# Top-32 attention and a Mish MLP in fp32: four engine programs turned from slots of one duo into rounds of four duos

## What is computed

```python
# q, k, v: (4, 8, 576, 64); w_in: (512, 2048); w_out: (2048, 512)
scores = scale * np.matmul(q, k.transpose(0, 1, 3, 2))
kth = np.partition(scores, -32, axis=-1)[..., -32:-32 + 1]
scores = np.where(scores >= kth, scores, -1000000000.0)
scores = scores - np.max(scores, axis=-1, keepdims=True)
attn = np.exp(scores)
attn = attn / (np.sum(attn, axis=-1, keepdims=True) + 1e-09)
x = np.matmul(attn, v).transpose(0, 2, 1, 3).reshape(2304, 512)
h = x @ w_in
y = (h * np.tanh(np.log1p(np.exp(h)))) @ w_out      # Mish, with h cut at 20 in the exponent
```

## Time and profile before

| what | value |
|---|---|
| median of 3 runs (lowest, highest) | 774.0 us (773.94, 775.21) |
| profiled execution: its time, its span | 774.75 us, 773.0 us |
| busy in the span: PE, DVE, ACT, POOL | 718.6, 700.3, 583.5, 547.0 us |
| longest instructions in sum | DVE `topk` MAX8 L574, 432 of 751 ns; PE `up` L388, 2304 records of 279 ns |
| DMA | 34.64 MB, mean 45 GB/s |

### The profile page before, as it was taken

One profiled execution on the slowest core, in us unless ns is written; L12 is line 12 of the kernel. 1 busy time (PEld: TensorE's weight loads), 2 busy tenths in 40 slices (PEclk: granted clock), 3 DMA queues, 4 the chain that ended last, 5 costly groups with the idle time before them and its releaser, 6 DMA issues.

```text
span 773.0 us, 16774 instructions
## 1 busy us (share of the span) xinstructions
PE 718.6 (93%) x6280; PEld 642.3 (83%) x6280; DVE 700.3 (91%) x1513; ACT 583.5 (75%) x1026; POOL 547.0 (71%) x677
## 2 busy tenths in 40 slices
PE   3266699999999999999999999999999999999998
PEld 2255688988888888888888888898899888888986
DVE  6999999999999999999999999999999999999000
ACT  5676677878787878888888888877888888887521
POOL 3877677798777777788777777778777777776531
PEclk9998989999999999999999999999999999999999
DMA  9521000031121000110110000011122000000000
GB/s 341 195 63 35 8 8 12 28 86 59 51 86 51 22 8 22 39 45 16 56 43 21 8 23 8 29 45 52 42 90 77 22 8 22 8 18 2 15 1 28
DMA packets 22689, 34.64 MB, mean 45 GB/s; under 512 B 2384, under 2 KB 11600, under 8 KB 22096
## 3 DMA queue, kind: packets, MB, share of 16 engines
q1 hardware_dynamic: 22608, 33.56, 13.3%
HBM read 28.84 MB, written 4.72 MB: 43 GB/s over the span
## 4 chain that ended last, share of the span: by engine, by line
PE 55%; DVE 35%; POOL 4%; issue 3%; ACT 3%; DMA 0%; SPq 0%; ACTq 0%
PE ps_u L388 22%; DVE left L566 17%; PE ps_y L401 16%; DVE top L574 13%; PE ps_s L329 5%; PE ps_s L347 5%; DVE top L559 5%; PE ps_o L372 5%; PE ps_o L365 1%; POOL g_lo L611 1%; POOL p_sb L625 1%; POOL p_sb L636 1%; ACT p_sb L472 1%; ACT L472 0%; ACT k_hi L432 0%
## 5 line engine op out<-in xcount | busy, mean ns | idle before, releaser
L574 DVE MAX8 top<-left 128x8 f32<-128x576 f32 x432 | 305.3, 751 | 0.0
L388 PE MATMUL ps_u<-xT,win 128*128 128x128 f32 x2304 | 276.6, 279 | 2.5 <-ACT xT L489 2.5
L388 PEld LDWEIGHTS ps_u<-xT,win 128*128 128x128 f32 x2304 | 264.9, 193 | 13.0 <-issue 8.4
L566 DVE MATCH_REPLACE8 left<-top,left 128x576 f32<-128x576 f32 x288 | 212.5, 749 | 0.0
L625 POOL TENSOR_TENSOR p_sb<-x_sb,p_sb 128x576 f32<-128x576 f32 x144 | 200.9, 1417 | 0.0
L472 ACT ACTIVATE p_sb<-p_sb,neg_max 128x576 f32<-128x576 f32 x144 | 110.7, 773 | 24.0 <-POOL p_sb L625 23.5
L453 ACT ACTIVATE x_sb<-ps_s 128x576 f32<-128x576 f32 x144 | 85.7, 648 | 46.1 <-PE ps_s L329 46.1
L401 PE MATMUL ps_y<-w_hi,g_hi 128*128 128x512 f32 x288 | 119.5, 415 | 0.0
L401 PE MATMUL ps_y<-w_hi,g_lo 128*128 128x512 f32 x288 | 113.1, 393 | 0.0
L401 PE MATMUL ps_y<-w_lo,g_hi 128*128 128x512 f32 x288 | 112.4, 390 | 0.0
L636 POOL TENSOR_SCALAR p_sb<-p_sb,recip 128x576 f32<-128x576 f32 x144 | 106.2, 749 | 8.3 <-DVE recip L549 8.0
(11 more groups left out here) (41 smaller groups left out, 823.5 us busy)
## 6 DMA issues: line engine op xcount, KB each, us to landing
v_sb<-v_in SPq DMA_DIRECT2D x32, 320.0 KB, 3.9
g_raw<-w_out SPq DMA_DIRECT2D x8, 512.0 KB, 3.9
win<-w_in SPq DMA_DIRECT2D x4, 1024.0 KB, 12.8
y_out<-y_sb SPq DMA_DIRECT2D x16, 256.0 KB, 2.0
k_raw<-k_in SPq DMA_DIRECT2D x14, 288.0 KB, 3.0
q_raw<-q_in SPq DMA_DIRECT2D x60, 64.0 KB, 1.8
q_raw<-q_in SPq DMA_DIRECT2D x8, 128.0 KB, 2.0
p_sb<-k_in SPq DMA_DIRECT2D x2, 288.0 KB, 5.3
```

The lines of the kernel that those rows point to most:

```text
L388: mm = pe.matmul(ps_u[:, n % 2, i, :], win[:, k, P * f:P * f + P], xT[:, k, :], start=(k == 0), stop=(k == KC - 1), skip_group_check=True)
L566: dve.match_replace(out=left[:, t, :], in_to_replace=best[:, t, EIGHT * r:EIGHT * r + EIGHT], in_values=x[t] if r == 0 else left[:, t, :], ...
L574: dve.max(best[:, t, EIGHT * r + EIGHT:EIGHT * r + 2 * EIGHT], left[:, t, :]).then_inc(found, 1)
```

## The change

Every engine's loop now runs over rounds of four duos, m from -2, with all steps of a round written out. In round m stand the steps of the duos 4m+4 to 4m+7 from `penalty` on, and both the whole `up` and the whole `down` of block m. The list differs from the slots in these points:
- block m's `down` stands in the same round as its `up`, where before it stood four slots later;
- on ACT, copies, penalties and exps are single steps in a new order; `copy_pT` stands between the exps of duos 4m+5 and 4m+6, and behind both of duo 4m+7;
- on DVE, `inverse(s - 2)` stands behind the first MAX8 of an odd duo, and behind the first MATCH_REPLACE8 of an even one;
- on POOL, the steps of g's split are two helpers; `negate`, `guard`, `normalise` and the splits stand in a new order, and the two subtractions of duo 4m+7 have a split of q between them;
- `exp` no longer waits on `negmax_ready`; the table load that the compiler puts ahead of the first exp after a Mish then has no wait of its own, where it had the wait on `arg_ready` before.

```diff
-LAG_EXP, LAG_NORM, LAG_PT = 1, 2, 3
+LAG_NORM = 2
-UP_SLOT, MISH_SLOT, DOWN_SLOT = 6, 8, 10
-SLOTS = DOWN_SLOT + DUOS
+FIRST_ROUND = -2
...
         def _(pe):
-            for s in range(-2, SLOTS):
-                if LAG_PT <= s < DUOS + LAG_PT:
-                    transposes(s - LAG_PT)
-                m, j = group_at(s, DOWN_SLOT)
-                if m is not None:
-                    down(m, j)
-                for d in (s - LAG_PT - 1, s - LAG_PT):
-                    if 0 <= d < DUOS and values_slot(d) == s:
-                        values(d)
-                if s + 2 < DUOS:
-                    scores(s + 2)
-                m, j = group_at(s, UP_SLOT)
-                if m is not None:
-                    up(m, j)
+            for m in range(FIRST_ROUND, BLOCKS):
+                values(4 * m + 2)
+                values(4 * m + 3)
+                scores(4 * m + 7)
+                up(m, 0)
+                transposes(4 * m + 4)
+                up(m, 1)
+                scores(4 * m + 8)
+                up(m, 2)
+                transposes(4 * m + 5)
+                up(m, 3)
+                scores(4 * m + 9)
+                values(4 * m + 4)
+                values(4 * m + 5)
+                transposes(4 * m + 6)
+                down(m, 0)
+                down(m, 1)
+                scores(4 * m + 10)
+                down(m, 2)
+                transposes(4 * m + 7)
+                down(m, 3)
...
-            def exps(s):
-                act.wait_ge(negmax_ready, s + 1)
-                for t in range(2):
-                    act.wait_ge(arg_ready, 2 * s + t + 1)
+            def exp(s, t):
+                act.wait_ge(arg_ready, 2 * s + t + 1)
...
+            for m in range(FIRST_ROUND, BLOCKS + 1):
+                splits(4 * m + 4)
+                penalty(4 * m + 4, 0)
+                copy_pT(4 * m + 3, 0)
+                copy_pT(4 * m + 3, 1)
+                penalty(4 * m + 4, 1)
+                exp(4 * m + 4, 0)
+                split_q(4 * m + 8)
+                exp(4 * m + 4, 1)
+                copy_xT(m)
+                penalty(4 * m + 5, 0)
+                penalty(4 * m + 5, 1)
+                copy_x(4 * m + 7, 0)
+                copy_x(4 * m + 7, 1)
+                split_q(4 * m + 9)
+                splits(4 * m + 5)
+                exp(4 * m + 5, 0)
+                copy_pT(4 * m + 4, 0)
+                exp(4 * m + 5, 1)
+                copy_pT(4 * m + 4, 1)
+                copy_up(m, 0)
+                copy_y(m - 1)
+                penalty(4 * m + 6, 0)
+                penalty(4 * m + 6, 1)
+                copy_up(m, 1)
+                copy_x(4 * m + 8, 0)
+                copy_x(4 * m + 8, 1)
+                splits(4 * m + 6)
+                mish(m, 0)
+                exp(4 * m + 6, 0)
+                copy_pT(4 * m + 5, 0)
+                copy_pT(4 * m + 5, 1)
+                exp(4 * m + 6, 1)
+                copy_up(m, 2)
+                split_q(4 * m + 10)
+                copy_up(m, 3)
+                penalty(4 * m + 7, 0)
+                copy_x(4 * m + 9, 0)
+                copy_x(4 * m + 9, 1)
+                penalty(4 * m + 7, 1)
+                mish(m, 1)
+                exp(4 * m + 7, 0)
+                exp(4 * m + 7, 1)
+                splits(4 * m + 7)
+                copy_pT(4 * m + 6, 0)
+                copy_pT(4 * m + 6, 1)
+                split_q(4 * m + 11)
+                copy_x(4 * m + 10, 0)
+                copy_x(4 * m + 10, 1)
...
                 for t in range(2):
+                    if s % 2 == 1 and t == 1:
+                        inverse(s - LAG_NORM)
                     dve.wait_ge(x_copied, 2 * s + t + 1)
                     dve.max(best[:, t, 0:EIGHT], x[t]).then_inc(top8_ready, 1)
                 for r in range(TOPK // EIGHT - 1):
                     for t in range(2):
+                        if s % 2 == 0 and r == 0 and t == 1:
+                            inverse(s - LAG_NORM)
...
-                    if r == 0 and s >= LAG_NORM:
-                        inverse(s - LAG_NORM)
...
+            for m in range(FIRST_ROUND, BLOCKS):
+                negate(4 * m + 4)
+                splits(4 * m + 4)
+                exponent(4 * m + 4, 0)
+                exponent(4 * m + 4, 1)
+                negate(4 * m + 5)
+                split_q(4 * m + 8)
+                guard(4 * m + 4)
+                normalise(4 * m + 4)
+                exponent(4 * m + 5, 0)
+                exponent(4 * m + 5, 1)
+                splits(4 * m + 5)
+                guard(4 * m + 5)
+                negate(4 * m + 6)
+                normalise(4 * m + 5)
+                exponent(4 * m + 6, 0)
+                exponent(4 * m + 6, 1)
+                splits(4 * m + 6)
+                split_g_hi(m, 0)
+                split_q(4 * m + 9)
+                split_g_lo(m, 0)
+                guard(4 * m + 6)
+                negate(4 * m + 7)
+                normalise(4 * m + 6)
+                exponent(4 * m + 7, 0)
+                split_q(4 * m + 10)
+                exponent(4 * m + 7, 1)
+                split_g_hi(m, 1)
+                split_g_lo(m, 1)
+                guard(4 * m + 7)
+                split_q(4 * m + 11)
+                normalise(4 * m + 7)
+                splits(4 * m + 7)
```

More of the change, by code:

```diff
@@ L107, with in_duos, in_blocks @@
 STAGED = PPB
[L110 to L119, removed]
+def in_duos(s):
+    return 0 <= s < DUOS
+def in_blocks(m):
+    return 0 <= m < BLOCKS
 def w_chunks_at(s):
@@ L377, in up @@
             def up(m, j):
+                if not in_blocks(m):
+                    return
                 n = GROUPS * m + j
@@ L434, in split_q @@
             def split_q(s):
+                if not 0 < s < DUOS:
+                    return
                 if s < STAGED:
@@ new lines, in exp, with copy_pT @@
+            def exp(s, t):
+                if not in_duos(s):
+                    return
+                act.wait_ge(arg_ready, 2 * s + t + 1)
+                p = p_sb[:, s % PS_, t, :]
+                act.activation(p, p, ACT.Exp, bias=neg_max[:, s % TS, t:t + 1], scale=SCALE,
+                               accum_out=denom[:, s % TS, t:t + 1]).then_inc(exp_ready, 1)
+            def copy_pT(s, i):
+                if not in_duos(s):
+                    return
+                if s >= 2 and i == 0:
@@ L514, in _ @@
             split_k(0)
-            split_q(0)
+            act.wait_ge(q_staged, 16)
+            act.activation(q_hi[:, 0, 0:P], q_source(0), ACT.Copy).then_inc(qhi_ready, 1)
             split_k(1)
-            for s in range(-2, SLOTS):
-                if LAG_PT <= s < DUOS + LAG_PT:
-                    copy_pT(s - LAG_PT)
-                if 0 <= s - LAG_EXP < DUOS:
-                    penalties(s - LAG_EXP)
-                if s + 3 < DUOS:
-                    split_q(s + 3)
-                m, j = group_at(s, UP_SLOT + 1)
-                if m is not None:
-                    copy_up(m, j)
-                if LAG_PT <= s < DUOS + LAG_PT and (s - LAG_PT) % PPB == PPB - 1:
-                    copy_xT((s - LAG_PT) // PPB)
-                if 0 <= s + 2 < DUOS:
-                    copy_x(s + 2)
-                m, j = group_at(s, DOWN_SLOT)
-                if m is not None and j == GROUPS - 1:
-                    copy_y(m)
-                if 0 <= s - LAG_EXP < DUOS:
-                    exps(s - LAG_EXP)
-                if s > -2:
-                    for g in splits_at(s):
-                        split_k(g)
-                for c in w_chunks_at(s):
-                    split_w(c)
-                m, h = half_at(s, MISH_SLOT)
-                if m is not None:
-                    mish(m, h)
@@ L601, in split_w, with splits, split_g_hi @@
                                    ALU.subtract).then_inc(wlo_ready, 1)
-            def split_g(m, h):
+            def splits(s):
+                for g in splits_at(s):
+                    split_k(g)
+                for c in w_chunks_at(s):
+                    split_w(c)
+            def split_g_hi(m, h):
+                if not in_blocks(m):
+                    return
                 f = slice(FT // 2 * h, FT // 2 * h + FT // 2)
```

184 lines of the change are left out of this document (108 added, 76 removed).

## The result

The changed kernel takes 776.49 us (median of 14 runs, 775.05 to 777.93), the kernel before in the same comparison 774.5 us. The ratio is 1.0023, with a 95% interval of 1.0015 to 1.0031: slower by 0.2%, where 763.6 us and 1.4% faster were forecast. The profiled execution has a span of 774.8 us, against 773.0.

The account below looks back on a forecast made before the run. DVE was taken to set the pace, PE close behind: body 707.46 us + stops 7.8 + tail 47.4 = 762.7 span; 764.4 with the 1.75 around it, less 0.75 for the median: 763.6. Range 757 to 773.

Parts of the forecast that it names:

- What bounds the kernel: DVE sets the pace at 9.71 us a duo; PE, at 9.68, has 0.03 us a duo in hand.
- the tail: From the end of DVE's last MAX8 (T) to the span's end: 47.4 us against 58.84, 11.4 us less.
- The rival of a bound PE: Each round: new matmul neighbours make PE's round 39.36 us, adding 3.6 us, 767.2 in all; chance 0.12.
- The ordinary stop: Duo 4m+7: POOL's list of 8.64 us exceeds DVE's 8.33, so DVE stops 0.31 us in each round.
- 0.55 forecast for round 0: Chunk 7 of w_out, in the same place as the double k splits, stops DVE for 0.55 us.
- The k rounds: Rounds 2 and 11: two k splits on POOL between duo 4m+6's subtractions and g_hi cost 1.6 us each round.
- SP's q loads: On SP: duo 4m+9's load can go at 10.9, is wanted at 13.9, others have more slack; costs nothing.
- exp without its second wait: On ACT: costs and brings nothing, as both subtractions are done when mish ends; if late, 1.28 us a load.
- The table load: Rival: three loads a round hold ACT longer than their row, giving 807 or about 812 us; chance 0.03.
- The late ACT as a rival: ACT, waiting in order for PE, is late in each of 16 rounds; 1.0 us late gives 779.6; chance 0.15.
- the forecast's signs for an ordinary round and for the tail: Wrong if DVE stops over 0.9 us in an ordinary round, PE's round exceeds 39.2, or tail exceeds 50.

Follow-up runs that it names:

- Run 3: Changed kernel with guard(4m+7) moved ahead of split_g_lo(m, 1) on POOL; 774.32 us, ratio 0.9994 to the kernel before.
- 8: Changed kernel with SP's order changed, k splits of slot 4m+7 last on ACT, and guard(4m+7) ahead of split_g_lo(m, 1); 765.65 us, ratio 0.9887.
- 10: Changed kernel with DVE's reciprocal back in its old place, behind the first pair of MATCH_REPLACE8 in each duo; 774.58 us, ratio 1.0000.
- 11: Changed kernel with SP's order changed, k splits of slot 4m+7 last on ACT, and the reciprocal in its old place; 765.53 us, ratio 0.9881.
- run 7: Changed kernel with the wait on negmax_ready put back ahead of exp; 776.09 us, ratio 1.0019 to the kernel before.
- run 4: Kernel before, with only exp's wait on negmax_ready removed; 771.95 us, ratio 0.9961.
- 1: Changed kernel, SP's order only: load_q(4m+9) ahead of v and k loads, a round's k loads ahead of q loads of duos 4m+10, 4m+11; 767.97 us.
- edits 1 and 2: On the changed kernel: SP issues k loads and load_q(4m+9) earlier (alone 767.97 us); k splits of slot 4m+7 go last on ACT (alone 767.14 us).
- run 9: Changed kernel with SP's order changed and the k splits of slot 4m+7 last on ACT, POOL untouched; 765.54 us, ratio 0.9885.

## Why the prediction was wrong, point by point

- **What bounds the kernel, and the tail: right.** 47.4 us forecast behind T, 47.04 measured; the pieces were the ones named. The rival of a bound PE did not decide in the changed kernel. It shows in runs 3 and 8, where DVE stops less, PE waits for g_lo and the tail grows by 2.1 and 1.7 us. The 1.3 us that the tail grows in 10 and 11 are something else: there PE still waits for POOL (0.76 us at 718.97 in 11). POOL's list starts later with the later reciprocal, and so its last normalise ends later.
- **The ordinary stop: right.** 0.31 forecast, 0.34 to 0.37 measured in nine of twelve rounds, for the reason given; 0.55 forecast for round 0, 0.58 measured (at 96.70). Run 3 takes it away by moving the guard, runs 10 and 11 by moving the point where it is wanted.
- **The overlap lost at a stop: missing.** I counted idle time alone. It is 0.11 us a stop, 1.8 us.
- **The k rounds: this step failed.** The prediction gave "1.6 us in each of these rounds" for the work of the splits between the subtractions and g_hi. That part measured 0.43 + 0.91 and 0.46 + 0.91, 1.3 to 1.4. But it stopped there. The other pair of k splits, of slot 4m+7, stands on ACT ahead of `copy_pT(4m+6)` and the split of q, and on POOL normalise stands behind that split of q. I had asked only whether they have the time, not what stands behind them if their data come late. Nor did the sum have the clock, which fell while PE stood behind them. The stops also came later than the forecast said, at 167 to 220 and 527 to 581 us, not near 130 to 150 and 480 to 500.
- **"SP's q loads [...] Nothing": the step behind it.** I went through the q loads in an ordinary round, and left out the k and v loads of the two batch changes. SP issues in order too: the k load stood behind two q loads with waits and 640 KB of v, 9.9 us after its buffer was free. From the double splits to the end of the round after them the stops are 3.05 + 1.01 + 0.90 + 4.59 + 1.31 = 10.9 us. The last of each bunch (0.90 and 1.31) stands where an ordinary stop of 0.31 was forecast, so 10.2 us are beyond the forecast, of the 12.1 us by which the span missed (774.8 against 762.7).
- **exp without its second wait: right for the new order** (run 7), where it stands behind mish with its data ready. In the order before it is worth 2.7 us (run 4), which the prediction did not claim either way.
- **The table load** holds ACT for its own 1.28 us and no more: in 69 of the changed kernel's 70 loads ACTIVATE starts 1.29 or 1.30 us after the load does (as 171.13 behind 169.84), so that rival falls. The one left is the first, 2.98 us.
- **The late ACT as a rival** was the nearest to what came: ACT in order behind a wait. It waited for a transfer first and for PE behind it, and in two places of the program, not in every round. None of the forecast's signs for an ordinary round and for the tail came (stops over 0.9 us, a tail over 50 us): they did not look at the rounds that failed.

The run that tells most is 1: no instruction of PE, DVE, ACT or POOL differs from the changed kernel, and it is 8.5 us faster. With edits 1 and 2 the new rounds give 765.5 us, 1.15% faster than the kernel before, near the 763.6 of the forecast. The last 1.9 us can be told from the numbers of run 9: its span is 763.6 against 762.7 (1.1 us lost beside the idle time with 13 more stops, 0.2 of idle time, the tail 0.4 shorter), and its median is 1.9 us above its span, where the forecast had added 1.75 and taken 0.75 away. Why the stops that were taken away beyond that (8, 11) brought nothing is only in part traced: in 8 the wait comes back on PE, in 11 in the tail and in stops of 1.1 to 1.8 us.

## What to carry to other kernels

When a loop is rolled out by hand over several engines, the steady round is only half of the layout: go through the rare steps (a new batch's loads and splits) with the same care, on the queue that issues transfers too, and ask of each wait what stands behind it in order. A load should be issued when its buffer comes free, not where its turn comes in a list whose other entries wait for later things. And put the work that waits for a rare load last among what is ready, so that its lateness costs only itself.

## What the runs showed of the hardware

- A stop cost DVE more than its idle time: 0.11 us more at an ordinary stop (39.26 us for a round with 0.35 idle, 38.80 for four duos without). Some of it is the overlap of neighbours: a MAX8 is 0.74 us long, and the next instruction starts 0.66 after it did (176.41 and 177.07 in the changed kernel).
- With one wait ahead of the ACTIVATE, the table load ran during the wait (run 4). With two the load itself waited (1.37 us at 616.03 in the earlier trace rows) and ran behind. That cost the kernel before 2.7 us (run 4), and the new order nothing (run 7).
- In rounds 2 and 11, after PE had stood for 2.6 to 3.8 us, its granted clock was 0.50 for 3.4 to 6.8 us although it was busy; where it stood 1.6 us at most it stayed at 1.00. So a wait cost PE more than its own length: 12 matmuls of the scores took 3.02 us in place of 1.71.
